# Activation of the first MoE written to SBUF by VectorE, its low part made by GpSimd

## What is computed

```python
# first MoE, x is the recurrence's output, w_in 384 x 2048, w_out 2048 x 384
h = x @ w_in
g = np.where(h >= 1, h, np.where(h <= -1, 0.0, (h + 1) ** 2 / 4))
x = g @ w_out
# second MoE: gate by exp and eight rounds of row and column scaling, then
for e in range(8):
    out += P[:, e:e + 1] * (np.maximum(x @ w1[e], 0.0) @ w2[e])
```

## Time and profile before

| | |
|---|---|
| median of 3 runs | 2386.37 us (2386.13 to 2387.14) |
| the profiled execution | 2386.86 us, its span 2385.1 us |
| PE, DVE, ACT, POOL busy | 95%, 65%, 41%, 19% of the span |
| mean granted clock of TensorE | 0.989 |

### The profile page before, as it was taken

How to read it: one execution, slowest core, us unless ns; L and a number is a source line. 1 busy time by engine, 2 the same in 40 slices (tenths; PEclk the granted TensorE clock), 3 DMA queues, 4 the chain that set the end, 5 groups by cost and what they waited for, 6 DMA issues and landing times.

```text
span 2385.1 us, 43991 instructions
## 1 busy us (share of the span) xinstructions
PE 2261.7 (95%) x16891; PEld 2241.0 (94%) x16891; DVE 1559.6 (65%) x2953; ACT 981.6 (41%) x1675; POOL 461.0 (19%) x325
## 2 busy tenths in 40 slices
PE   2689999999999989999999999999999999999999
PEld 2689999999999889999999999999999999999999
DVE  6898888888874685555556666555556655565553
ACT  2455555555555433333333433333333333333331
POOL 0000000000000312222222222122222222222221
PEclk9799999999999999999999999999999999999999
DMA  3211111111112310011112211110013211111101
GB/s 105 84 33 48 49 49 49 49 50 49 50 37 71 120 54 24 31 54 54 55 54 93 94 54 54 55 53 25 32 54 117 70 54 54 54 54 54 54 1 27
DMA packets 73194, 132.46 MB, mean 56 GB/s; under 512 B 5608, under 2 KB 36584, under 8 KB 72936
## 3 DMA queue, kind: packets, MB, share of 16 engines
q1 hardware_dynamic: 72936, 129.14, 16.4%
HBM read 114.96 MB, written 14.16 MB: 54 GB/s over the span
## 4 chain that ended last, share of the span: by engine, by line
PE 81%; DVE 10%; ACT 7%; issue 2%; DMA 0%; DVEq 0%; ACTq 0%; SPq 0%
PE bank L1431 13%; PE bank L1433 13%; PE bank L1432 13%; PE bank L1598 11%; PE bank L1599 11%; PE bank L1600 11%; PE bank L1412 2%; PE bank L1418 2%; PE bank L1417 2%; PE bank L1422 1%; ACT ubuf L648 1%; ACT ubuf L650 1%; PE bank L1407 1%; ACT ubuf L646 1%; DVE tmp L861 1%
## 5 line engine op out<-in xcount | busy, mean ns | idle before, releaser
L1431 PE MATMUL bank<-x_h,w_h 128*128 128x256 f32 x2112 | 595.8, 282 | 9.0 <-issue 4.1
L1433 PE MATMUL bank<-x_h,w_l 128*128 128x256 f32 x2112 | 595.0, 282 | 0.0
L1432 PE MATMUL bank<-x_l,w_h 128*128 128x256 f32 x2112 | 594.1, 281 | 0.0
L1598 PE MATMUL bank<-w_h,h_h 128*128 128x384 f32 x1536 | 518.2, 337 | 0.4 <-DVE acc L1233 0.4
L1600 PE MATMUL bank<-w_h,h_l 128*128 128x384 f32 x1536 | 515.0, 335 | 0.0
L1599 PE MATMUL bank<-w_l,h_h 128*128 128x384 f32 x1536 | 514.9, 335 | 0.0
L567 POOL TENSOR_TENSOR h_l<-u_s,h_h 128x512 fp32r<-128x512 f32 x192 | 244.6, 1295 | 1136.6 <-ACT h_h L778 1136.6
L1431 PEld LDWEIGHTS bank<-x_h,w_h 128*128 128x128 f32 x2112 | 400.7, 190 | 11.9 <-issue 6.0
L1432 PEld LDWEIGHTS bank<-x_l,w_h 128*128 128x128 f32 x2112 | 401.9, 190 | 0.0
L1433 PEld LDWEIGHTS bank<-x_h,w_l 128*128 128x128 f32 x2112 | 401.5, 190 | 0.0
L1240 DVE SCALAR_TENSOR_TENSOR acc<-bank,prob,acc 128x384 f32<-128x384 f32 x168 | 103.5, 616 | 370.6 <-PE bank L1600 370.6
(11 more groups left out here) (164 smaller groups left out, 4035.8 us busy)
## 6 DMA issues: line engine op xcount, KB each, us to landing
stage<-w_ SPq DMA_DIRECT2D x48, 768.0 KB, 7.9
w_raw<-w_ SPq DMA_DIRECT2D x96, 384.0 KB, 4.8
qb<-q_in_ SPq DMA_DIRECT2D x24, 192.0 KB
kb<-k_in_ SPq DMA_DIRECT2D x24, 192.0 KB
vb<-v_in_ SPq DMA_DIRECT2D x24, 192.0 KB
x_hi<-x2h_s SPq DMA_DIRECT2D x36, 128.0 KB, 1.8
x_lo<-x2l_s SPq DMA_DIRECT2D x36, 128.0 KB, 1.8
x_h<-x_hi SPq DMA_DIRECT2D x6, 768.0 KB, 4.4
```

Source lines behind the costliest of these rows:

```text
L1431: pe.matmul(dst, w[0], x[0], start=first, stop=False)
L1432: pe.matmul(dst, w[0], x[1], start=False, stop=False)
L1433: return pe.matmul(dst, w[1], x[0], start=False, stop=last)
L1598: pe.matmul(dst, h_h[:, f, t_], w2s[slot][0][:, f], start=n == 0, stop=False)
```

## The change

g_max writes g to `ubuf` in SBUF instead of back to the bank. ScalarE's g_hi reads it there. g_lo moves from VectorE to GpSimd, reads `ubuf`, and keeps its four places a unit, now in GpSimd's queue among `check_y` and `pre_inv`; `pre_inv(u)` is issued at the beginning of unit u behind g_lo(t-1), no longer at the end of unit u - 1. `mm_in(t)` now waits for g_max(t - 2), and `g_sq(t)` for g_lo(t - 2).

```diff
--- before.py
+++ after.py
@@ -551,10 +551,25 @@
                 with pool.If(bits > R_BITS):
                     recurrence(u)
 
+            def g_lo(t):
+                pool.wait_ge(gh_done, t + 1)
+                pool.tensor_tensor(g_l[:, t % 2], ubuf[:, t % 2], g_h[:, t % 2].bitcast(F32), ALU.subtract)\
+                    .then_inc(gl_done, 1)
+
             for u in range(UNITS):
+                t = 4 * (u - 2) - 1
+                if u > 2:
+                    g_lo(t - 1)
+                if u >= 2:
+                    pre_inv(u)
+                if u > 2:
+                    g_lo(t)
                 check_y(u)
-                if 2 <= u + 1 < UNITS:
-                    pre_inv(u + 1)
+                if u >= 2:
+                    g_lo(t + 1)
+                    g_lo(t + 2)
+            for t in range((GROUPS - 1) * TILES - 2, GROUPS * TILES):
+                g_lo(t)
 
             def w2_lo(ex, slot, lo=0, hi=NW2):
                 for i in range(lo, hi):
@@ -641,7 +656,7 @@
 
                 act.wait_ge(h_full, t + 1)
                 if t >= 2:
-                    act.wait_ge(g_done, t - 1)
+                    act.wait_ge(gl_done, t - 1)
                 buf = ubuf[:, t % 2]
                 act.activation(buf, hb[t % 2][:], ACT.Relu, bias=0.5, scale=-0.5).then_inc(w_done, 1)
                 act.wait_ge(w_done, t + 1)
@@ -653,7 +668,7 @@
                 act.wait_ge(g_done, t + 1)
                 if t >= 2:
                     act.wait_ge(out1_done, t - 1)
-                act.activation(g_h[:, t % 2], hb[t % 2][:], ACT.Copy).then_inc(gh_done, 1)
+                act.activation(g_h[:, t % 2], ubuf[:, t % 2], ACT.Copy).then_inc(gh_done, 1)
 
             def x2_hi(c):
                 act.wait_ge(out1_done, (c + 1) * TILES)
@@ -992,12 +1007,7 @@
 
             def g_max(t):
                 dve.wait_ge(sq_done, t + 1)
-                dve.tensor_tensor(hb[t % 2][:], hb[t % 2][:], ubuf[:, t % 2], ALU.max).then_inc(g_done, 1)
-
-            def g_lo(t):
-                dve.wait_ge(gh_done, t + 1)
-                dve.tensor_tensor(g_l[:, t % 2], hb[t % 2][:], g_h[:, t % 2].bitcast(F32), ALU.subtract)\
-                   .then_inc(gl_done, 1)
+                dve.tensor_tensor(ubuf[:, t % 2], hb[t % 2][:], ubuf[:, t % 2], ALU.max).then_inc(g_done, 1)
 
             def x2_lo(c):
                 for n in range(KT):
@@ -1042,8 +1052,6 @@
                 more = u + 1 < UNITS
                 pair = u // 2 + 1
                 scans = not even and more
-                if u > 2:
-                    g_lo(t - 1)
                 if not even and u >= 5:
                     gate_out(u // 2 - 2)
                 by_qk(u, 0)
@@ -1056,8 +1064,6 @@
                 if scans:
                     blocks(pair, 1, 5)
                 by_qk(u, 1)
-                if u > 2:
-                    g_lo(t)
                 if moe:
                     g_max(t + 1)
                 if even:
@@ -1072,7 +1078,6 @@
                 if u < 4:
                     first_lo(SPLIT_AT[2 * u], SPLIT_AT[2 * u + 1])
                 if moe:
-                    g_lo(t + 1)
                     g_max(t + 2)
                 if even:
                     p_inv(u + 1)
@@ -1083,8 +1088,6 @@
                 state_add(u)
                 if even and u >= 4:
                     x2_lo(u // 2 - 2)
-                if moe:
-                    g_lo(t + 2)
                 if scans:
                     final(u + 1)
                 if moe:
@@ -1190,7 +1192,6 @@
                     w1_sums(0, 1)
                 if m == 6:
                     w1_lo(0, 1)
-            g_lo(GROUPS * TILES - 1)
             x2_lo(GROUPS - 1)
 
             def add(g, name, product, kept):
@@ -1439,7 +1440,7 @@
                 if g == 0:
                     pe.wait_ge(piece_l, PIECES.index((0, m)) + 1)
                 if t >= 2:
-                    pe.wait_ge(gl_done, t - 1)
+                    pe.wait_ge(g_done, t - 1)
                 for a in range(2):
                     c_ = slice((2 * m + a) * 128, (2 * m + a + 1) * 128)
                     for kk in range(KT):
```

## The result

The changed kernel takes 2439.43 us in the median of four runs (2436.38 to 2441.41), the kernel before 2386.25 us (2384.96 to 2387.14) beside it: a ratio of 1.0222, 95% interval 1.0204 to 1.024, so 2.2% slower. The forecast was 2428 us, range 2400 to 2446. The profiled execution took 2436.38 us (the fastest of the four), its span 2434.6 us at a mean granted clock of 0.981.

The account below looks back on a forecast made before the run. TensorE was taken to bound the kernel, with waits for qt and ks to win; 4.05 us a pair times ten gave 40.5, plus 1.5 elsewhere, so 2386.4 + 42 = 2428 us, range 2400 to 2446.

Parts of the forecast that it names:

- The lock: VectorE instructions with two SBUF inputs stand until the running GpSimd instruction is within 0.14 us of its end.
- Rival (a): VectorE's back-to-back instructions keep the ports and GpSimd starts only in its pauses: 2380 us, chance 12%.
- cost GpSimd nothing: Short VectorE instructions slip in at the seams between GpSimd's four w_l's, which still took 7.23 us.
- a subtraction well beyond 1.3 us: Sign of being wrong: GpSimd's subtractions stretched well beyond 1.3 us would mean the lock is shared out otherwise.
- its 0.14 us: How far before the running GpSimd instruction's end a held VectorE instruction seems to start.
- Odd head, +1.95: At odd units' start, GpSimd's g_lo and pinv make scale() 2.55 us late, less 0.60 for g_lo: +1.95 us a pair.
- the longer of the forecast's two cases: At the odd head GpSimd holds the ports to about 484.6 us, first letting two of VectorE's instructions finish.
- Rival (b): Only one block at the odd head, pre_inv slipping behind scale(): 2.05 us a pair, 2407 us, chance 15%.
- Even unit, +0.65: On the path to ks, pinv behind g_lo makes final's first product 0.57 us late: +0.65 us a pair in all.
- Odd body with the clock, +1.15 and +0.3: GpSimd's g_lo delays blocks(), kt and mask, +1.15 us a pair; clock falls at about half the odd heads, +0.3.
- Relief alone, 10 x 0.6: Taking g_lo off VectorE gains 0.6 us at each of ten odd heads, 6 us; nothing at even heads.

Follow-up runs that it names:

- pre_inv early: The changed kernel with GpSimd's product pinv back at the end of the unit before, g_lo still on GpSimd: 2410.3 us, 1.01.
- g_lo behind qt: The kernel before with VectorE's g_lo(t-1) moved from ahead of qt to behind it, nothing moved to GpSimd: 2388.65 us, 1.0009.
- ks first on the changed kernel: The changed kernel with ScalarE copying ks ahead of p_root in even units: 2457.09 us, 1.0296.
- g_lo of one column: The changed kernel with pinv issued early and GpSimd's g_lo subtracting one column of 512 from its third tile on: 2386.32 us, 1.0003.
- the memset: The changed kernel with pinv issued early and GpSimd's g_lo replaced by a memset of g_l, without input: 2381.78 us, 0.9982.
- one column and pinv late: The changed kernel, pinv left behind g_lo(t-1), with g_lo subtracting one column of 512 from its third tile on: 2407.64 us, 1.0089.

## Why the prediction was right

**The lock (step "what comes onto GpSimd").** Shown. The blocked instructions are those within SBUF, for as long as GpSimd's runs, and the loss goes when that instruction is short or only writes (2410.3 to 2386.32 and 2381.78). Rival (a), GpSimd gives way, falls: it stands for 0.15 to 0.3 us, only for what is left of an instruction that VectorE has begun, and holds VectorE for 0.4 to 1.5. The forecast left this out ("cost GpSimd nothing") and named a subtraction well beyond 1.3 us as a sign of being wrong; at the odd heads it is 1.59, by the same lock. The held products end 0.41 us behind GpSimd's instruction, as in the forecast's row, so its 0.14 us stands.

**Odd head, +1.95.** Measured +1.9 to 2.1. As written, g_lo and pinv join, and scale's second and third instruction stand to their ends. Together the two last 3.7 us, the longer of the forecast's two cases. Rival (b), one block only, is what pre_inv early gives; its 2407 stands beside 2410.3.

**Even unit, +0.65.** L933 is 0.57 us longer, held by pinv behind g_lo as forecast, and the path's three waits change by -0.97, +0.82 and +0.66: +0.5.

**Odd body with the clock, +1.15 and +0.3.** In the seven of nine pairs whose odd head is followed by a fall, kt comes 7.3 to 7.6 us behind the head where it was 5.9 to 6.0, some +1.5 in all, and neither kt nor the mask is waited for; in the two others they are, 0.6 and 0.25 us, and the mask's matmul comes 1.2 us later. Over the nine that is 1.45, as forecast, but in part by luck: falls follow more heads than the half that I took, and each adds less than the 0.55 I gave it.

**The term that was mis-sized: the clock.** From odd head to odd head the changed kernel takes 63.3 to 63.7 us in six of eight intervals, +4.2 on 59.33 against +4.05 forecast, and 64.9 in two. Those two have a fall behind the wait for ks of 1.60 us, which the forecast had priced as a wait and not as a fall: 1.4 us each over the other six, 2.7 of the 4.0 us by which the eight intervals pass the forecast. Other runs show such falls: they make a pair 1.6 us longer with g_lo behind qt, and cost ks first on the changed kernel its 18 us.

**The rest.** Of the 49.5 us by which the span grew, 9.0 lie ahead of the first odd head at 198 us (7.0 forecast), 36.4 in the eight pairs (32.4), 4.1 behind (2.6; the wait for x2l_s grew by 0.5). Ahead of that head TensorE stands at the low clock for 41.0 us where it was 34.1, which the forecast hadn't priced either. The profiled execution was the fastest; its 2436.38 is 8 us over the forecast, the median 11. Of the 3 us between them no trace is kept, but the mean granted clock of the three slower executions is 0.976 to 0.979 and that of the profiled one 0.981. A share of 0.002 of 2437 us is 5 us of the clock, so more falls are likely; where they lie isn't shown.

**Relief alone, 10 x 0.6.** The pair gives it, as the runs with g_lo of one column and with the memset show (odd head 0.92 to 0.54, a pair 58.7, -0.6). The 6 us for the kernel came in none of them: -4.3 us with the memset, nothing with the one column. The first units part these two, 24 and 41 us at half clock.

**Left open:** why a wait of 1.6 us for ks is followed by a fall in some pairs and not in others of the same kernel; and the time at half clock in the first units, 20 to 41 us over these kernels, which I can't derive from their waits.

## What to carry to other kernels

An elementwise instruction that reads SBUF, moved to GpSimd, can cost its old neighbours on VectorE that work within SBUF GpSimd's duration, not VectorE's: here, pinv's move included, eight times 0.60 us saved a pair against 6.5 us of hold. Before moving work off an engine, list what runs beside it on the other that reads SBUF twice, and try first whether a step in front of the critical one can go behind it: three such swaps together gave 14 us where the move cost 53. And when one wait is shortened, look which wait becomes longest: behind some of 1.5 us and more TensorE's clock fell here, behind those of 1.25 us in the kernel before it never did.

## What was unexpected of the hardware

In the pairs a wait of 1.25 us on TensorE was never followed by a low clock in the trace of before; one of 1.48 to 1.60 us sometimes (three pairs with g_lo behind qt, two in the changed kernel), one of 2.8 to 3.0 us in seven of nine; the granted clock is then 0.58 to 0.61 over the next 3.4 to 3.6 us, level 1.2 GHz for most of it. The length isn't all: of the odd heads' waits of 1.97 to 2.19 us, with one column and pinv late, only one of nine was. With the wait of 1.77 us for the mask it stayed low for up to 10.2 us: the price of a fall isn't fixed. And the lock holds GpSimd too. Its subtraction went from 1.30 to 1.59 us and its product from 1.82 to 2.16 where an instruction of VectorE's scale had 0.46 us to go as they started. In that stretch without a break the engines took turns, one instruction each, and VectorE stood longer because GpSimd's were the longer ones.
